# Dividing the columns of each sequence as 482, 512 and 512 in place of three chunks of 502

## The reference

```python
x = real(fft(fft(x, axis=1), axis=2))      # x: 2 x 3008 x 256, both transforms full
x = x.reshape(6016, 256)
h = x @ w_in                               # 256 -> 2048
x = (h * sigmoid(h)) @ w_out               # 2048 -> 256
h = x @ w2_in                              # 256 -> 2048
y = (max(h, 0) + alpha * min(h, 0)) @ w2_out   # 2048 -> 256
```

## Time and profile before

| | us |
|---|---|
| runs | 933.08, 934.04, 954.89 |
| median | 934.04 |
| the profiled execution, its own time | 933.09 |
| span of its trace | 931.2 |
| granted clock of PE, mean | 0.999 |

### The profile page before, as it was taken

How to read it: one execution, slowest core, us unless ns; L and a number is a source line. 1 busy time by engine, 2 the same in 40 slices (tenths; PEclk the granted TensorE clock), 3 DMA queues, 4 the chain that set the end, 5 groups by cost and what they waited for, 6 DMA issues and landing times.

```text
span 931.2 us, 11837 instructions
## 1 busy us (share of the span) xinstructions
PE 923.3 (99%) x4034; PEld 757.2 (81%) x4034; DVE 635.2 (68%) x967; ACT 551.6 (59%) x858; POOL 594.4 (64%) x408
## 2 busy tenths in 40 slices
PE   9999999999999999999999999999999999999998
PEld 4588887788888888888888888888888888888886
DVE  6879996455545545544877777777777777778774
ACT  4575654567667656676665565465555555555544
POOL 0496555259959859676697476566747756664443
PEclk9999999999999999999999999999999999999999
DMA  9512100020020120100300200020020002001001
GB/s 361 222 56 68 45 1 1 1 67 23 13 78 23 55 80 1 45 1 1 124 11 1 71 20 1 0 89 1 1 88 1 1 1 89 1 1 44 1 1 45
DMA packets 19826, 40.35 MB, mean 43 GB/s; under 512 B 1803, under 2 KB 15669, under 8 KB 18741
## 3 DMA queue, kind: packets, MB, share of 16 engines
q1 hardware_dynamic: 18980, 39.05, 11.9%
q10 hardware_dynamic: 688, 0.52, 0.2%
q0 software_dynamic: 96, 0.02, 0.0%
HBM read 27.22 MB, written 12.37 MB: 43 GB/s over the span
## 4 chain that ended last, share of the span: by engine, by line
PE 94%; DVE 2%; POOL 1%; DMA 1%; ACT 1%; issue 0%; SPq 0%; DVEq 0%; ACTq 0%; POOLq 0%
PE ps L354 12%; PE ps L352 12%; PE ps L353 12%; PE ps L668 9%; PE ps L671 9%; PE ps L667 9%; PE ps L613 9%; PE ps L609 9%; PE ps L610 9%; DMA x_tile<-x_tiles 1%; PE ps L556 1%; POOL gl L1313 1%; PE ps L541 1%; PE ps L537 1%; POOL wo L1248 0%
## 5 line engine op out<-in xcount | busy, mean ns | idle before, releaser
L1335 POOL TENSOR_TENSOR gl<-g,gh 128x502 fp32r<-128x502 f32 x192 | 224.8, 1178 | 175.3 <-ACT gh L857 175.3
L1313 POOL TENSOR_TENSOR gl<-g_sb,gh 128x1004 fp32r<-128x1004 f32 x96 | 210.3, 2190 | 121.2 <-ACT g_sb L814 119.2
L851 ACT ACTIVATE g<-ps 128x502 f32<-128x502 f32 x192 | 111.9, 591 | 110.3 <-DVE ps L1196 105.3
L1148 DVE SCALAR_TENSOR_TENSOR h_sb<-n_all,a,v_sb 128x502 f32<-128x502 f32 x96 | 83.1, 865 | 135.1 <-ACT v_sb L876 135.0
L1203 DVE SCALAR_TENSOR_TENSOR g<-g,less_alpha,ps 128x502 f32<-128x502 f32 x192 | 132.6, 732 | 31.9 <-ACT g L851 31.8
L609 PE MATMUL ps<-gh,wo 128*128 128x502 f32 x384 | 148.8, 388 | 0.3
L610 PE MATMUL ps<-gh,wo 128*128 128x502 f32 x384 | 147.9, 385 | 0.0
L667 PE MATMUL ps<-gh,wo 128*128 128x502 f32 x382 | 147.3, 386 | 0.0
L668 PE MATMUL ps<-gh,wo 128*128 128x502 f32 x382 | 147.3, 386 | 0.0
L857 ACT CAST gh<-g 128x502 fp32r<-128x502 f32 x192 | 113.0, 614 | 40.3 <-DVE g L1203 38.6
L876 ACT COPY v_sb<-ps 128x502 f32<-128x502 f32 x96 | 55.6, 580 | 122.5 <-PE ps L354 118.4
(11 more groups left out here) (132 smaller groups left out, 1618.4 us busy)
## 6 DMA issues: line engine op xcount, KB each, us to landing
x_tile<-x_tiles SPq DMA_DIRECT2D x6, 1024.0 KB, 13.5
x_rows<-x SPq DMA_DIRECT2D x6, 1004.0 KB, 5.9
out_t<-out_sb SPq DMA_DIRECT2D x11, 502.0 KB, 3.2
x_raw_b<-x_rows SPq DMA_DIRECT2D x18, 251.0 KB, 4.0
stage<-moe_w_out SPq DMA_DIRECT2D x16, 256.0 KB, 4.5
n_parts<-n_rows SPq DMA_DIRECT2D x5, 502.0 KB, 3.7
stage<-moe_w_in SPq DMA_DIRECT2D x8, 256.0 KB, 5.0
w_sb<-moe_w_in SPq DMA_DIRECT2D x3, 512.0 KB, 7.8
```

The costliest lines, as they stand in the source:

```text
L851: act.activation(g4[:, k, :], product_bank(u, TILE_IN[k]), ACT.Relu, scale=-1.0).then_inc(relu_done, 1)
L1313: pool.tensor_tensor(gl[g % 2][:, :, :], g_sb[g % 2][:, :, :], gh[g % 2][:, :, :].bitcast(F32), ALU.subtract).then_inc(gl_done, 1)
L1335: pool.tensor_tensor(gl4[:, k, :], g4[:, k, :], gh4[:, k, :].bitcast(F32), ALU.subtract).then_inc(gl_done, 1)
```

## The change

The chunks of each sequence get the widths 482, 512 and 512. `N` is gone: `WIDTHS` holds the width and `STARTS` the first column of each chunk, and every view and copy takes the width of its chunk. There are still six chunks, 96 steps and 48 units, so the number of matmuls stays. All buffers are 512 columns wide, and the offsets of those that were 2016 bytes apart become multiples of 2048. In DRAM, `x1_rows` has rows of 512 columns, `out_t` becomes one row of all columns for each feature, and `n_rows` is stored by one DMA for each chunk (5 in all, 4 before). The pieces that `cut` gives stay as many: block 1 is divided after 106 of its columns (126 before), block 2 after 242 (252 before). The columns of the transform itself, 376 and 378, do not change.

```diff
-N = COLS // 3
 ROW = 512
-NC1 = 3 * BATCH
-NC2 = 2 * NC1
+NC0 = -(-COLS // ROW)
+NC1 = BATCH * NC0
+WIDTHS = ([COLS - ROW * (NC0 - 1)] + [ROW] * (NC0 - 1)) * BATCH
+STARTS = [sum(WIDTHS[:c]) for c in range(NC1 + 1)]
...
-        h_sb = [at(f"h_sb{i}", OPA_AT + (4032, 12288)[i], [P, 2, N], F32) for i in range(2)]
-        n_parts = at("n_parts", OPA_AT + 8192, [P, 2, N], F32)
-        g_sb = [at(f"g_sb{i}", OPA_AT + 16320 + W2N * i, [P, 2, N], F32) for i in range(2)]
+        h_sb = [at(f"h_sb{i}", OPA_AT + (4096, 12288)[i], [P, 2, ROW], F32) for i in range(2)]
+        n_parts = at("n_parts", OPA_AT + 8192, [P, 2, ROW], F32)
+        g_sb = [at(f"g_sb{i}", OPA_AT + 16384 + W2R * i, [P, 2, ROW], F32) for i in range(2)]
...
-            return ps[:, bank:bank + 2, 0:N]
+            return ps[:, bank:bank + 2, 0:WIDTHS[g // NF]]
...
-            return ps[:, (7 * u + list(PRODUCTS).index(p) + pair_at(STEPS1 - 2)) % 4, 0:N]
+            return ps[:, (7 * u + list(PRODUCTS).index(p) + pair_at(STEPS1 - 2)) % 4, 0:WIDTHS[u // HF]]
...
-                for i in range(2):
-                    sp.dma_start(n_rows[first:last, i * N:(i + 1) * N].rearrange("(a c) t -> a c t", a=1),
-                                 pq[0:1, first:last, 2 + i, :].bitcast(F32)).then_inc(n_out, 16)
+                for c in range(first, last):
+                    wd = WIDTHS[c]
+                    sp.dma_start(n_rows[c:c + 1, 0:2 * wd].rearrange("c (i t) -> c i t", i=2),
+                                 pq[0:1, c, 2:4, 0:wd].bitcast(F32)).then_inc(n_out, 16)
...
-                    if c in (4, 5):
+                    if c >= 3:
                         pe.wait_ge(t23_lo, len(T23_JOBS))
-                three(pe, u, ab[:, 0, 0, fs], ab[:, 0, 1, fs], pq[:, c, 0, :], pq[:, c, 1, :], True, True)
-                three(pe, v, ab[:, 1, 0, fs], ab[:, 1, 1, fs], pq[:, c, 2, :], pq[:, c, 3, :],
-                      True, True).then_inc(mm1, 1)
+                p_hi, p_lo, q_hi, q_lo = (pq[:, c, i, 0:WIDTHS[c]] for i in range(4))
+                three(pe, u, ab[:, 0, 0, fs], ab[:, 0, 1, fs], p_hi, p_lo, True, True)
+                three(pe, v, ab[:, 1, 0, fs], ab[:, 1, 1, fs], q_hi, q_lo, True, True).then_inc(mm1, 1)
...
-                    pe.matmul(dst, wh, gh[g % 2][:, sg, :], start=f == 0, stop=False)
+                    pe.matmul(dst, wh, gh[g % 2][:, sg, 0:WIDTHS[c]], start=f == 0, stop=False)
...
-                xh, xl = (xr[n % 2][x, i][:, :] for i in range(2))
+                xh, xl = (xr[n % 2][x, i][:, 0:WIDTHS[n]] for i in range(2))
...
-                pool.tensor_tensor(gl[g % 2][:, :, :], g_sb[g % 2][:, :, :], gh[g % 2][:, :, :].bitcast(F32),
-                                   ALU.subtract).then_inc(gl_done, 1)
+                g_lo, g_raw, g_hi = (t[g % 2][:, :, 0:WIDTHS[g // NF]] for t in (gl, g_sb, gh))
+                pool.tensor_tensor(g_lo, g_raw, g_hi.bitcast(F32), ALU.subtract).then_inc(gl_done, 1)
...
-    out_t = nc.dram_tensor("out_t", (D, NC2, N), F32, kind="ExternalOutput").ap()
+    out_t = nc.dram_tensor("out_t", (D, 2 * BATCH * COLS), F32, kind="ExternalOutput").ap()
```

More of the change, by code:

```diff
@@ L42, with cut @@
 JOB_AFTER = {1: "n", 28: "t1p", 29: "t1q", 30: "t2", 31: "t3"}
[L45 to L51, removed]
+def cut(b, blk):
+    at, out, done = b * COLS + BLOCK_AT[blk], [], 0
+    while done < BLOCK_W[blk]:
+        c = max(i for i in range(NC1) if STARTS[i] <= at + done)
+        w = min(BLOCK_W[blk] - done, STARTS[c + 1] - at - done)
+        out.append((c, at + done - STARTS[c], done, w))
         done += w
@@ L153, in build @@
         assert XS_AT + 8192 + 2 * ROW * 4 <= STAGE_AT and W1_AT + 14 * ROW * 4 <= W2_AT
-        xr = [{row: at(f"x_{row[0]}_{row[1]}_{i}", place, [P, N], F32R) for row, place in X_PLACE[i].items()} for i in range(2)]
-        xr_raw = [{x: at(f"x_raw_{x}_{i}", X_PLACE[i][x, 1], [P, N], F32) for x in X_ROWS} for i in range(2)]
+        xr = [{row: at(f"x_{row[0]}_{row[1]}_{i}", place, [P, ROW], F32R) for row, place in X_PLACE[i].items()} for i in range(2)]
+        xr_raw = [{x: at(f"x_raw_{x}_{i}", X_PLACE[i][x, 1], [P, ROW], F32) for x in X_ROWS} for i in range(2)]
         stage = [at(f"stage{i}", STAGE_AT + 2048 * i, [P, 512], F32) for i in range(SLOTS)]
@@ L601, in second1 @@
                     pe.wait_ge(stage_lo, f // 2 + 1)
-                out = [(sg, ft, ps[:, 4 + 2 * sg + ft, 0:N]) for sg in range(2) for ft in range(2)]
+                out = [(sg, ft, ps[:, 4 + 2 * sg + ft, 0:WIDTHS[c]]) for sg in range(2) for ft in range(2)]
                 for sg, ft, dst in out:
@@ L657, in second2 @@
                 pe.wait_ge(gh_done, STEPS1 + 4 * u + k + 1)
-                out = [ps[:, 4 + 2 * sg + ft, 0:N] for ft in range(2)]
+                out = [ps[:, 4 + 2 * sg + ft, 0:WIDTHS[n]] for ft in range(2)]
+                g_hi, g_lo = (t[:, k, 0:WIDTHS[n]] for t in (gh4, gl4))
                 if (u, k) == (UNITS - 1, 3):
@@ L1092, in t23_low @@
                 bank = t_bank(blk, b, s)
[L1093 removed]
+                for c, o, a, w in cut(b or 0, blk):
                     if s == "n":
@@ L1193, in half_sum @@
                     dve.wait_ge(comb, 7 * u + (-1, 1, 1, 3, 3, 3, 3)[i])
-                add = p1_sb[:, :] if other is None else h3[:, other, :]
+                wd = WIDTHS[u // HF]
+                add = p1_sb[:, 0:wd] if other is None else h3[:, other, 0:wd]
                 bank = product_bank(u, p)
-                dve.tensor_tensor(h3[:, i, :] if i < 3 else bank, bank, add, ALU.add).then_inc(comb, 1)
+                dve.tensor_tensor(h3[:, i, 0:wd] if i < 3 else bank, bank, add, ALU.add).then_inc(comb, 1)
             def prelu(u, k):
@@ L1428, in token_columns @@
                 sign = 1 - sign
-            c, o = divmod(b * COLS + at[k], N)
-            idx[b, s] = (2 * c + sign) * N + o
+            j = b * COLS + at[k]
+            c = max(i for i in range(NC1) if STARTS[i] <= j)
+            idx[b, s] = STARTS[c] + sign * WIDTHS[c] + j
     return idx.reshape(-1)
```

164 lines of the change are left out of this document (87 added, 77 removed).

## The result

| | us |
|---|---|
| after, median of 4 runs | 939.99 (939.87 to 940.11) |
| before, median of 4 runs (the three of the first table and one more) | 934.64 |
| ratio of their undisturbed runs | 1.0067, 95% interval 1.0051 to 1.0083 |
| the profiled execution after, its own time | 939.97, span 938.1 |

The change makes the kernel slower by 0.7%, 6.3 us by the ratio; the two spans differ by 6.9 us. The forecast was no change, 934, with a range from 925 to 945. (One run of before in the first table, 954.89, is a disturbed one and left out of the ratio.)

What follows compares the result with a forecast made beforehand. It took PE, at its own pace, to bound the kernel. Pitches 0, chunk 0 steps +0.2, PE's first steps -0.2, last output +0.01 and offsets 0 summed to 0: forecast 934 us, range 925 to 945.

Steps and rivals of the forecast that it cites:

- The sum over pitches: PE's 3888 matmuls: 1296 at 215.0 ns plus 2592 at 227.5 make 868.3 us, a change of 0.
- the floor: PE's pitch can't go below about 223.3 ns: 482 columns gain nothing, 512 pay 4.2 ns, 945 us; chance 0.06.
- I take the same for fp32r: pitch = columns / 2.4 + 14.1: PE's fp32r matmuls: a fixed remainder at every width, as in plain fp32; 215.0 ns at 482, 227.5 at 512.
- the line: PE's fp32r pitch taken as columns / 2.4 + 14.1 ns: 215.0 at 482 columns, 227.5 at 512.
- The excess of 14.1 ns belongs to a width that doesn't fill the row: First rival, PE: 512 columns would keep only 2.2 ns of excess, 215.5 ns in all; 903 us; chance 0.08.
- Rounding to 16: Weaker form of the first rival: PE's columns round up to 16, giving 496, 512, 512; 925 us; chance 0.07.
- The second term: the offsets, "-0.5 to +1 us, take 0": New offsets of ACT, DVE and POOL buffers: bounded from PE's 3.1 us of waits for POOL, taken as 0.
- The forecast of 4.22 us for these steps: Chunk 0's four steps without a POOL gap: 4.33 us falls to 4.22, where PE could do 3.87.
- third rival: Steps of chunks 0 and 3 stay engine-bound at 4.02 us: 32 x 0.15 = +4.8, 939 us; chance 0.03.

Runs made afterwards that it cites:

- e_move64: The kernel before, with everything from `W1_AT` on 64 bytes further in SBUF and nothing else changed: 944.82 us, ratio 1.0114.

## Why the prediction was wrong

**What held.** PE is the bound, the count of 3888 matmuls, full clock, nothing slower on ACT, stage 2 without waits, and nothing from the DMAs. The sum over pitches was the right way to count; the terms in it were wrong. That 940 lies inside the range is luck: the upper end, 945, came from the floor, which isn't there.

**The step that failed: "I take the same for fp32r: pitch = columns / 2.4 + 14.1".** 512 came out at 226.7 for the 227.5 of the line, -2.2 us, and 482 at 220.0 for 215.0, +6.5 us; together the +4.3. The argument for it was that the remainder doesn't step with the width in plain fp32, where a record makes two passes. Those records stay at about 2 ns over their columns; fp32r has 13.3 to 22.7 and moves with the width by more than the 8.3 ns that the change takes off the columns, so that the one can't stand for the other. The measured pitch of one width can't tell whether that width is a good one. 502 is: of the widths tried above 440, only 500, 502, 510 and 512 stay within 2 ns of the least excess.

**The rivals.** "The excess of 14.1 ns belongs to a width that doesn't fill the row" is out: 512 has the least excess near 502, but it is 13.4 and not 2.2, and 502 has nearly the same. Rounding to 16 is out by 498 and 500. The second, the floor, had the right sign and the right chunk for the loss (482 gives little back, and 9.90 us a unit isn't the 10.05 of a full floor), and the wrong cause: 256 columns take 120 ns. It priced 945 with 482 at 223.3 and 512 at the line; the pitches measured give 938.

**The second term: the offsets, "-0.5 to +1 us, take 0".** They cost 2.5 us. The bound was drawn from PE's waits for POOL, as if these could only change in proportion; and I wrote that no row had the same operation at another offset. Row for row it was there: the timeline of stage 2 has `gl` of 128x502 at 1.08 and at 1.28 us in turn, and the prediction doesn't ask why. It also passes over the steps at which POOL adds n, 4.25 us before and so already over PE's 4.02, where nearly half of the 2.6 us came in. In chunk 0, where POOL has no gap, each 0.1 us of a subtraction goes into the step. The forecast of 4.22 us for these steps became 4.38 to 4.41.

**The steps bound by an engine (third rival).** Not at 4.02 and not in 32 steps: the narrow steps without extra work ran at 3.96, PE's own pace, and only those with extra work were bound by POOL.

## What to carry to other kernels

Where PE is the bound, take the pitch of fp32r matmuls at each width from a run, before dividing work into other widths: between 480 and 512 columns it runs from 216.6 to 227.5 ns (508 columns), not in order of width, and it depends on the place of the operands: 64 bytes on part of them cost a kernel of the same widths 1.1%. Moving a buffer by some bytes is not free of effects: check the matmuls, those whose operands stay as well, and the two-input operations of POOL whose inputs come into step. Even a gain there can be lost again: a POOL instruction that ends sooner lets the next one start sooner, and it can meet a DVE instruction it didn't meet before (0.74 us became 1.73). And look at one instruction's durations one by one, since a mean of 1178 ns was made of 1.07 and 1.28.

## What the hardware did that I had not expected

PE: fp32r matmuls of 128 stationary columns, back to back at full clock, take columns / 2.4 ns plus 13.3 at best (256, 384 and 512 columns, the two operands a multiple of 256 bytes apart), 22.7 at 488. At 16 of the 20 widths the pitch averages to a multiple of 3.33 ns, within 0.1. With one operand 32 to 128 bytes off, 502 columns take 3.3 to 4.7 ns more and 512 2.2 to 6.8; with both 64 bytes off, nothing. What makes this is open: the runs show that place and width count, not the mechanism, and in `e_move64` matmuls slowed down whose own operands had stayed.

POOL: a subtraction of two inputs of 502 columns takes 1.242 us when both start at the same place within 16 bytes (or the first 4 bytes further), and 1.07 to 1.08 when they are 8 bytes apart (or the second 4 bytes further, or the first 12); moving the output by 8 bytes changes nothing.
